# Ranking the second unit of a slot one operation behind the first, in a fused attention and feed-forward kernel

## The chip, the cores and the metric

The kernel runs on one core of a Trainium2 chip. The metric is the device time of one execution in microseconds; the median of three runs before the change is 1221.03 us (1220.47 to 1221.56).

## The reference

Attention that keeps, for each query, only the scores that reach the 32nd largest, then two feed-forward layers of different kind on the result. Batch 4, 8 heads, 576 tokens, 64 dimensions a head; 2304 tokens of 512 features, 2048 hidden.

```python
scores = scale * q @ k^T                       # 4 x 8 x 576 x 576
kth = the 32nd largest of each row
scores = where(scores >= kth, scores, -1e9)
attn = exp(scores - max); attn = attn / (sum(attn) + 1e-9)
x = (attn @ v), heads side by side             # 2304 x 512
h = x @ w_in                                   # first layer
g = h where h >= 1, 0 where h <= -1, else (h + 1)^2 / 4
x = g @ w_out
h = max(x @ w_in2, 0)                          # second layer
out = (h * h) @ w_out2
```

## The kernel before

Attention is cut into units: one head's 128 queries against all 576 keys. Two units make a slot `n`, t = 0 and t = 1 (two heads of the same rows); slots 0 to 63 hold the full blocks, 64 to 71 the packed tails. Matmuls of float32 accuracy are made of three with rounded halves: a value is split into a rounded part (`hi`, by ScalarE) and a rest (`lo`, by GpSimd or VectorE).

A unit goes through the engines in this order. TensorE makes its scores (`score`, L605) and ScalarE copies them to one of four buffers `s_sb` (`copy_scores`, L814), which waits until the masked product of four units before is made. VectorE ranks (`rank`, L1080): four MAX8 (L1086), each giving the next eight largest, with three MATCH_REPLACE8 (L1088) between that strike them out; `RANK_OPS` is 7. ScalarE negates the maxima of both units in one instruction (`negate`, L822) and makes the exponentials (`exponentiate`, L835). The mask comes from the 32nd value: in slots below `SIGNED` = 9 ScalarE makes it with two sign instructions (`keep_by_sign`, L853 and L856), later GpSimd (L1270); GpSimd multiplies it with the exponentials (L1275). TensorE turns the product (`turn_main`, L632), ScalarE copies it (`copy_main`, L863, `copy_shared`, L868), TensorE multiplies by v (`times_v`, L654 and L659) with a column of ones that gives the sum. VectorE takes the sum two slots later (`add_to_total`, L1094) and inverts it (L1104); ScalarE or VectorE scales the result into `x_nat` (L877).

Each engine runs a list of instructions that is written out by hand, slot by slot, and in order. In slot `n` ScalarE has first the signs of slot n-1, then the negation and first exponential of slot n, the scores of slot n+1 and turned tiles of slot n-1 between the two exponentials and behind them, and at the end the rounding of weight blocks for the next slot (`split_ahead`, L801). GpSimd has the products of slot n-1, then the rest of a preparation (`split_kq`, L1253), then weight blocks (L1261). VectorE has for each of the seven operations the first unit and then the second, with other work at fixed operations.

A preparation splits k and q of a pair of heads: SP loads it (L389), ScalarE rounds it into `kq_hi` (L793), GpSimd makes `kq_lo` (L1253), and SP stores both to DRAM (`restack`, L397), from where the slots load `ks` and `qs` (L402, L409). `PREP_SLOT` puts them in slots 1, 3, 5, 7, then 10, 12, 14, 16 and later. Up to slot 17 ScalarE's rounding stands ahead of the second exponential; the loads that SP has in its list behind a `restack` or a weight block wait with it.

The feed-forward work fills TensorE in steps at positions q = 3n, 3n+1, 3n+2: an up product (L700), the curve in three ScalarE instructions and one of VectorE (L1149), the split into `g_hi` and `g_lo` (L974, L977, L1288), a down product (L728, L734) two positions later. It starts at position 31, in slot 10; slots 10 to 17 (`SINGLE`) have two steps, later ones three. After slot 73 only feed-forward work is left.

One semaphore, `rank_step`, counts the rank operations of both units, two per operation.

Of the kernel before, what the change touches and what calls it, by code (L numbers as in the profile page):

```python
# [187 lines left out]
def build(nc, kq, kq0, vv, w_raw, out):  # L188
# [8 lines left out]
    with ctx:  # L197
# [64 lines left out]
        s_copied = sem("s_copied")  # L262
        rank_step = sem("rank_step")
        negated = sem("negated")
# [523 lines left out]
        def _(act):  # L788
# [28 lines left out]

            def negate(n):
                act.wait_ge(rank_step, 2 * RANK_OPS * n + 2)
                if n >= 2:  # L820
                    act.wait_ge(exp_done, 2 * n - 2)
                act.activation(neg_max[n % 2][:, :], top[n % 2][:, :, 0], ACT.Copy,  # L822
                               scale=-SCALE).then_inc(negated, 1)

            def exponentiate(n, t):
                i = (2 * n + t) % 4
                if t == 0:
                    act.wait_ge(negated, n + 1)
                    if n >= 2:
                        act.wait_ge(main_turned[1], n - 1)  # L830
                        act.wait_ge(shared_turned, n - 1)
# [15 lines left out]
            def keep_by_sign(n, t):  # L847

                u = 2 * n + t
                s = s_sb[u % 4]  # L850
                act.wait_ge(exp_done, u + 1)
                act.wait_ge(rank_step, 2 * RANK_OPS * (n + 1) - 1 + t)
                act.activation(s[:, :], s[:, :], ACT.Sign, bias=top[n % 2][:, t, TOPK - 1:TOPK],  # L853
                               scale=-1.0).then_inc(below, 1)
                act.wait_ge(below, u + 1)
                act.activation(s[:, :], s[:, :], ACT.Sign, bias=1.0, scale=-1.0).then_inc(keep_done, 1)  # L856
# [157 lines left out]
            def slot(n):  # L1014
# [13 lines left out]
                if here:  # L1028
                    negate(n)
                    exponentiate(n, 0)  # L1030
# [7 lines left out]
                if n in PREP_SLOT and n in SINGLE:  # L1038
                    hi_at(q)
                if n in SINGLE or q < UP_POS[0]:  # L1040
                    split_new(n)
                if here:
                    exponentiate(n, 1)
                if n in SCALED and n not in SINGLE:
# [9 lines left out]
                copy_at(q + 1)  # L1054
                hi_at(q + 1)
                split_ahead(n)
                if n > SINGLE[-1]:
# [18 lines left out]
        def _(dve):  # L1076
            def rank(n, t, op):
                i, done = (2 * n + t) % 4, op // 2
                src = s_sb[i] if done == 0 else rest[t]
                if op == 0:  # L1080
                    dve.wait_ge(s_copied, 2 * n + t + 1)
                else:
                    dve.wait_ge(rank_step, 2 * RANK_OPS * n + 2 * (op - 1) + t + 1)
                best = top[n % 2][:, t, 8 * done:8 * done + 8]
                if op % 2 == 0:
                    dve.max(best, src[:, :]).then_inc(rank_step, 1)  # L1086
                else:
                    dve.match_replace(rest[t][:, :], best, src[:, :], LOWEST).then_inc(rank_step, 1)  # L1088

# [100 lines left out]
            def slot(n):  # L1190
                here, past = n < SLOTS, 0 <= n - 2 < SLOTS and n - 2 not in SOON

                def both(op):
                    if here:
                        rank(n, 0, op)
                        rank(n, 1, op)

# [11 lines left out]
                for op in (2, 3, 4, 5, 6):  # L1209
# [6 lines left out]
                    if op == 4:  # L1216
                        read_at(3 * n + 1)
                        if n >= DEFERRED[0]:
                            activate_at(3 * n + 1)
                    if here:  # L1220
                        rank(n, 0, op)
                        if op == 2 and n in SINGLE:
                            invert_total(n - 2)
                        rank(n, 1, op)
                    if op == (3 if n in SINGLE and n - 1 in PREP_SLOT else 2):
# [24 lines left out]
        def _(pool):  # L1250
# [13 lines left out]
            def mask(n, t):  # L1264
                u = 2 * n + t
                s, pr = s_sb[u % 4], prob[n % 2]
                pool.wait_ge(exp_done, u + 1)
                pool.wait_ge(rank_step, 2 * RANK_OPS * (n + 1) - 1 + t)
                if n >= SIGNED:
# [121 lines left out]
```

## Time and profile before

| | |
|---|---|
| median of three runs | 1221.03 us (1220.47 to 1221.56) |
| profiled execution | 1220.98 us, span 1219.2 us |
| TensorE busy | 1174.0 us, 96% |
| VectorE busy | 833.0 us, 68% |
| ScalarE busy | 784.0 us, 64% |
| GpSimd busy | 740.3 us, 61% |

The shares are means over unlike stages. The first ten slots have no feed-forward work; the last third of the time has no attention. The span is counted from the first to the last instruction; the execution's time has some more around it.

### The profile page before, as it was taken

How to read it: one execution, taken by the hardware profiler on the slowest of the kernel's cores; microseconds unless marked ns; L12 is line 12 of the kernel's file. 1: busy time of each engine (PE TensorE's matmuls, PEld its weight loads, DVE VectorE, ACT ScalarE, POOL GpSimd, SP SyncE). 2: the span in 40 equal slices, each digit the busy share in tenths (PEclk: the TensorE clock that was granted, in tenths of full speed). 3: DMA queues.
4: the chain of work that ended last, by engine and by line, in shares of the span. 5: the costliest groups of instructions: out<-in, count | busy, mean ns of one | idle time of the engine just before them, and what ended most of it. 6: DMA issues, size and time to landing. Idle time of an engine off the chain costs nothing.

```text
span 1219.2 us, 22952 instructions
## 1 busy us (share of the span) xinstructions
PE 1174.0 (96%) x8120; PEld 1089.9 (89%) x8120; DVE 833.0 (68%) x1847; ACT 784.0 (64%) x1704; POOL 740.3 (61%) x589
## 2 busy tenths in 40 slices
PE   5878999999999999999999999999999999999998
PEld 3777899999889999999999999998999888998887
DVE  7999999999988799999999987878830211110000
ACT  7887777787656767767676665666554544653343
POOL 6777887888877677677776766666742222222222
PEclk9957999999999999999999999999999999999999
DMA  6777897678869923433458831567449400870000
GB/s 252 266 267 252 282 360 295 251 268 315 302 253 393 379 75 109 147 121 112 140 208 297 294 112 41 130 173 183 109 160 361 167 1 1 338 318 1 1 35 18
DMA packets 93377, 237.34 MB, mean 195 GB/s; under 512 B 10320, under 2 KB 45136, under 8 KB 80976
## 3 DMA queue, kind: packets, MB, share of 16 engines
q1 hardware_dynamic: 93104, 235.62, 54.9%
q8 instruction: 65, 1.06, 0.4%
q14 instruction: 48, 0.39, 0.1%
q10 hardware_dynamic: 160, 0.26, 0.1%
HBM read 164.02 MB, written 71.83 MB: 193 GB/s over the span
## 4 chain that ended last, share of the span: by engine, by line
PE 74%; DVE 9%; POOL 8%; ACT 4%; issue 3%; DMA 1%; SPq 0%; ACTq 0%; POOLq 0%; DVEq 0%
PE h_ps L700 22%; PE y_ps L728 11%; PE y_ps L734 10%; PE pv_ps L659 6%; PE score_ps L700 6%; DVE top L1086 5%; PE tr_ps L632 4%; DVE rest L1088 4%; PE score_ps L605 3%; POOL s_sb L1270 3%; POOL prob L1275 2%; POOL kq_lo L1253 2%; PE y_ps L720 2%; PE y_ps L723 2%; PE tr_ps L720 2%
## 5 line engine op out<-in xcount | busy, mean ns | idle before, releaser
L700 PE MATMUL h_ps<-xt_ks,w_in 128*128 128x256 f32 (+1 forms) x2628 | 384.5, 296 | 2.3 <-ACT rg L961 1.6
L700 PEld LDWEIGHTS h_ps<-xt_ks,w_in 128*128 128x128 f32 x2628 | 342.1, 191 | 12.8 <-ACT rg L961 2.0
L1288 POOL TENSOR_TENSOR g_lo<-rg,g_hi 128x256 fp32r<-128x256 f32 x224 | 169.4, 756 | 270.4 <-ACT g_hi L974 153.6
L1086 DVE MAX8 top<-rest 128x8 f32<-128x576 f32 x432 | 305.1, 746 | 0.4
L1270 POOL TENSOR_SCALAR s_sb<-s_sb,top 128x576 f32<-128x576 f32 x126 | 221.5, 1758 | 31.3 <-DVE top L1086 31.3
L1088 DVE MATCH_REPLACE8 rest<-top,rest 128x576 f32<-128x576 f32 x288 | 211.5, 741 | 0.0
L1275 POOL TENSOR_TENSOR prob<-s_sb,prob 128x576 f32<-128x576 f32 x128 | 182.9, 1431 | 16.3 <-ACT s_sb L856 3.5
L728 PE MATMUL y_ps<-g_hi,w_out 128*128 128x256 f32 x896 | 181.4, 285 | 0.6 <-POOL g_lo L1288 0.5
L734 PE MATMUL y_ps<-w_out,g_hi 128*128 128x512 f32 x448 | 158.5, 395 | 1.0 <-ACT moves L935 0.8
L728 PEld LDWEIGHTS y_ps<-g_hi,w_out 128*128 128x128 f32 x896 | 147.5, 191 | 2.1 <-POOL g_lo L1288 1.0
L659 PE MATMUL pv_ps<-v_sb,pt 128*128 128x65 f32 x1024 | 133.6, 288 | 0.0
L659 PEld LDWEIGHTS pv_ps<-v_sb,pt 128*128 128x128 f32 x1024 | 132.1, 209 | 0.0
L728 PE MATMUL y_ps<-g_lo,w_out 128*128 128x256 f32 x448 | 126.7, 283 | 0.0
L814 ACT ACTIVATE s_sb<-score_ps 128x576 f32<-128x576 f32 x143 | 92.1, 644 | 42.2 <-PE score_ps L605 23.4
L1086 DVE MAX8 top<-s_sb 128x8 f32<-128x576 f32 x144 | 102.4, 744 | 12.8 <-ACT s_sb L814 12.7
L632 PE MATMUL tr_ps<-ident,prob 128*128 128x128 f32 x576 | 93.6, 288 | 14.5 <-POOL prob L1275 14.2
L1088 DVE MATCH_REPLACE8 rest<-top,s_sb 128x576 f32<-128x576 f32 x144 | 105.7, 740 | 0.1
L1149 DVE SCALAR_TENSOR_TENSOR rg<-rg 128x256 f32<-128x256 f32 x112 | 59.5, 531 | 62.3 <-ACT rg L967 62.0
L835 ACT ACTIVATE prob<-s_sb,neg_max 128x576 f32<-128x576 f32 x128 | 99.4, 777 | 2.1
L734 PEld LDWEIGHTS y_ps<-w_out,g_hi 128*128 128x128 f32 x448 | 84.5, 189 | 17.7 <-issue 1.4
L956 ACT ACTIVATE rg<-h_ps 128x256 f32<-128x256 f32 x99 | 37.9, 383 | 88.9 <-PE h_ps L700 88.8
L605 PE MATMUL score_ps<-xt_ks,qs_g 128*128 128x288 f32 x480 | 90.9, 314 | 3.0 <-DMA qs_g<-kq_scratch 1.5
(117 smaller groups left out, 1821.8 us busy)
## 6 DMA issues: line engine op xcount, KB each, us to landing
w_in<-w_scratch SPq DMA_DIRECT2D x32, 1024.0 KB, 7.1
w_out<-w_scratch SPq DMA_DIRECT2D x32, 1024.0 KB, 8.4
xt_ks<-kq_scratch SPq DMA_DIRECT2D x30, 576.0 KB, 7.2
w_scratch<-w_in SPq DMA_DIRECT2D x16, 1024.0 KB, 7.2
w_scratch<-w_out SPq DMA_DIRECT2D x16, 1024.0 KB, 6.7
v_sb<-in_vv_dram SPq DMA_DIRECT2D x48, 325.0 KB, 6.1
qs_g<-kq_scratch SPq DMA_DIRECT2D x120, 128.0 KB, 4.3
moves<-in_w_dram SPq DMA_DIRECT2D x27, 512.0 KB, 5.9
```

The source lines that it names most:

```text
L605: last = pe.matmul(score_ps[:, 512 * half:512 * half + HALF], qq[:, t, var, :], kk[:, t, HALF * half:HALF * (half + 1)], start=(var == 0), ...
L632: last = pe.transpose(tr_ps[t][:, P * j:P * (j + 1)], prob[n % 2][:, base + P * j:base + P * (j + 1)], ident[:, :])
L659: last = pe.matmul(pv_ps[:, V1 * t:V1 * (t + 1)], pt[:, base + P * j:base + P * (j + 1)], vb[:, V1 * (2 * j + t):V1 * (2 * j + t + 1)], st ...
L700: last = pe.matmul(h_bank(k), wi[:, f // 2, w, m, cols], x_part(k, x, m), start=(m == 0 and n == 0), stop=(m == KT - 1 and n == 2))
L728: last = pe.matmul(y_ps[i][:, CHUNK * (m % 2):CHUNK * (m % 2 + 1)], wo[:, f // 2, w, f % 2, P * m:P * (m + 1)], g[f % 2][:, :], start=(f = ...
L734: last = pe.matmul(y_ps[i][:, :], g[f % 2][:, P * i:P * (i + 1)], wo[:, f // 2, w, f % 2, :], start=(f == 0 and n == 0), stop=(f == FT - 1 ...
L835: act.activation(pr[:, SEQ * t:SEQ * (t + 1)], s_sb[i][:, :], ACT.Exp, bias=bias[:, t:t + 1], scale=SCALE).then_inc(exp_done, 1)
L1086: dve.max(best, src[:, :]).then_inc(rank_step, 1)
L1088: dve.match_replace(rest[t][:, :], best, src[:, :], LOWEST).then_inc(rank_step, 1)
L1270: pool.tensor_scalar(s[:, :], s[:, :], top[n % 2][:, t, TOPK - 1:TOPK], None, ALU.is_ge).then_inc(keep_done, 1)
L1275: pool.tensor_tensor(pr[:, cols], s[:, :], pr[:, cols], ALU.mult).then_inc(masked, 1)
L1288: pool.tensor_tensor(lo_of(k), u_of(k), hi_of(k).bitcast(F32), ALU.subtract).then_inc(g_lo_done, 1)
```

## The change

- VectorE: the second unit's operation `op` - 1 stands where its operation `op` stood; its last operation stands behind the first operation of the next slot's first unit.
- `rank_step` becomes two semaphores, one for each unit, and all that wait for it wait for their unit's.
- ScalarE: `negate` works on one unit, 128x1 instead of 128x2. That of the second unit stands just ahead of the second exponential, and both exponentials wait for theirs.
- ScalarE: in slots 1, 3, 5 and 7 `split_new` (the rounding of a preparation) moves from ahead of the second exponential to the end of the slot, ahead of `split_ahead`. In slots 10 to 17 it stays.

```diff
-        rank_step = sem("rank_step")
+        rank_step = [sem(f"rank_step{i}") for i in range(2)]
...
-            def negate(n):
-                act.wait_ge(rank_step, 2 * RANK_OPS * n + 2)
+            def negate(n, t):
+                act.wait_ge(rank_step[t], RANK_OPS * n + 1)
                 if n >= 2:
                     act.wait_ge(exp_done, 2 * n - 2)
-                act.activation(neg_max[n % 2][:, :], top[n % 2][:, :, 0], ACT.Copy,
+                act.activation(neg_max[n % 2][:, t:t + 1], top[n % 2][:, t, 0:1], ACT.Copy,
                                scale=-SCALE).then_inc(negated, 1)
 
             def exponentiate(n, t):
                 i = (2 * n + t) % 4
+                act.wait_ge(negated, 2 * n + t + 1)
                 if t == 0:
-                    act.wait_ge(negated, n + 1)
...
                 if here:
-                    negate(n)
+                    negate(n, 0)
                     exponentiate(n, 0)
...
-                if n in SINGLE or q < UP_POS[0]:
+                if n in SINGLE:
                     split_new(n)
                 if here:
+                    negate(n, 1)
                     exponentiate(n, 1)
...
                 copy_at(q + 1)
                 hi_at(q + 1)
+                if n < SINGLE[0]:
+                    split_new(n)
                 split_ahead(n)
...
-                def both(op):
+                def first(op):
                     if here:
                         rank(n, 0, op)
-                        rank(n, 1, op)
+
+                def second(op):
+
+                    if op and here:
+                        rank(n, 1, op - 1)
+                    if op == 0 and 0 <= n - 1 < SLOTS:
+                        rank(n - 1, 1, RANK_OPS - 1)
+
+                def both(op):
+                    first(op)
+                    second(op)
...
-                    if here:
-                        rank(n, 0, op)
-                        if op == 2 and n in SINGLE:
-                            invert_total(n - 2)
-                        rank(n, 1, op)
+                    first(op)
+                    if op == 2 and n in SINGLE:
+                        invert_total(n - 2)
+                    second(op)
```

## Rows read from the trace of the kernel before

**Rows 1.** Busy time by stretch: PE, PEld, DVE, ACT, POOL, granted clock, DMA share, GB/s.

```profile
0.00:107.25 107.25, 80.30 (x319) 65.70 (x320) 98.03 (x216) 89.64 (x155) 77.25 (x46) 0.82 0.75 264
107.25:193.45 86.20, 80.53 (x635) 77.44 (x634) 84.95 (x194) 63.02 (x146) 71.70 (x51) 0.97 0.84 312
...
193.45:1219.20 1025.75, 1013.13 (x7170) 946.77 (x7168) 649.96 (x1439) 631.37 (x1404) 591.39 (x494) 1.00 0.51 177
...
77.95:97.49 19.54, 15.45 (x71) 14.04 (x70) 19.54 (x46) 18.43 (x34) 15.68 (x10) 0.63 0.76 277
```

**Rows 2.** Chain of waits, 76 to 106 us: shares by line.

```profile
by line: DVE top L1086 52.8%; DVE rest L1088 46.1%; DVE total L1094 0.6%; DVE recip L1104 0.6%
```

**Rows 3.** Timeline of ScalarE, slots 5 to 7: start, length, instruction [idle before].

```profile
65.97 1.21 ACT L793 ACTIVATE kq_hi<-kq_lo 128x1216 fp32r<-128x1216 f32 x1
67.08 0.77 ACT L835 ACTIVATE prob<-s_sb,neg_max 128x576 f32<-128x576 f32 x1
...
69.30 1.09 ACT L801 ACTIVATE w_out<-moves 128x1024 fp32r<-128x1024 f32 x1
...
71.20 0.81 ACT L853 ACTIVATE s_sb<-s_sb,top 128x576 f32<-128x576 f32 x1
...
74.01 0.19 ACT L822 ACTIVATE neg_max<-top 128x2 f32<-128x2 f32 x1
74.23 0.78 ACT L835 ACTIVATE prob<-s_sb,neg_max 128x576 f32<-128x576 f32 x1
74.91 0.63 ACT L814 ACTIVATE s_sb<-score_ps 128x576 f32<-128x576 f32 x1
75.58 0.60 ACT L863 ACTIVATE pt<-tr_ps 128x512 f32<-128x512 f32 x1
...
83.92 0.65 ACT L814 ACTIVATE s_sb<-score_ps 128x576 f32<-128x576 f32 x1 [0.74 <-POOL prob L1275]
...
90.43 0.81 ACT L853 ACTIVATE s_sb<-s_sb,top 128x576 f32<-128x576 f32 x1
```

**Rows 4.** Waits, 7 to 107 us: us in total, times, longest.

```profile
POOL kq_lo L1253 <- ACT kq_hi L793: 11.0, 4, 4.2
...
DVE top L1086 <- ACT s_sb L814: 8.7, 4, 7.1
```

**Rows 5.** Timeline of VectorE, slot 6: the second unit's first MAX8.

```profile
68.83 0.76 DVE L1086 MAX8 top<-s_sb 128x8 f32<-128x576 f32 x1 [0.94 <-ACT s_sb L814]
```

**Rows 6.** Timeline of ScalarE, end of slot 14.

```profile
161.27 0.28 ACT L868 ACTIVATE pt<-tr_ps 128x128 f32<-128x128 f32 x1
161.75 0.42 ACT L977 ACTIVATE g_hi<-rg 128x256 fp32r<-128x256 f32 x1 [0.21 <-DVE rg L1149]
```

**Rows 7.** Timeline of GpSimd, products of slot 1, then slots 5 and 6.

```profile
30.72 2.78 POOL L1275 TENSOR_TENSOR prob<-s_sb,prob 128x576 f32<-128x576 f32 x2 [0.58 <-ACT s_sb L856]
...
67.26 2.76 POOL L1253 TENSOR_TENSOR kq_lo<-kq_lo,kq_hi 128x1216 fp32r<-128x1216 f32 x1 [4.15 <-ACT kq_hi L793]
69.98 2.37 POOL L1261 TENSOR_TENSOR w_in<-moves,w_in 128x1024 fp32r<-128x1024 f32 x1
72.89 2.80 POOL L1275 TENSOR_TENSOR prob<-s_sb,prob 128x576 f32<-128x576 f32 x2 [0.54 <-ACT s_sb L856]
```

**Rows 8.** Timeline of TensorE: transposes, products with v, slots 6 and 8.

```profile
74.49 1.05 PE L632 MATMUL tr_ps<-ident,prob 128*128 128x128 f32 x4
...
79.24 3.52 PE L659 MATMUL pv_ps<-v_sb,pt 128*128 128x65 f32 x16
...
98.07 1.90 PE L659 MATMUL pv_ps<-v_sb,pt 128*128 128x65 f32 x16
```

**Rows 9.** Timeline of SP's issues, slots 3 and 4, and of TensorE's scores.

```profile
51.80 0.33 SPq L466 DMA_DIRECT2D moves<-in_w_dram  x1
...
57.38 1.24 SPq L409 DMA_DIRECT2D qs_g<-kq_scratch  x2
...
63.29 1.30 PE L605 MATMUL score_ps<-xt_ks,qs_g 128*128 128x288 f32 x4 [1.51 <-DMA qs_g<-kq_scratch]
```

More of the change, by code:

```diff
@@ L851, in keep_by_sign @@
                 act.wait_ge(exp_done, u + 1)
-                act.wait_ge(rank_step, 2 * RANK_OPS * (n + 1) - 1 + t)
+                act.wait_ge(rank_step[t], RANK_OPS * (n + 1))
                 act.activation(s[:, :], s[:, :], ACT.Sign, bias=top[n % 2][:, t, TOPK - 1:TOPK],
@@ L1082, in rank @@
                 else:
-                    dve.wait_ge(rank_step, 2 * RANK_OPS * n + 2 * (op - 1) + t + 1)
+                    dve.wait_ge(rank_step[t], RANK_OPS * n + op)
                 best = top[n % 2][:, t, 8 * done:8 * done + 8]
                 if op % 2 == 0:
-                    dve.max(best, src[:, :]).then_inc(rank_step, 1)
+                    dve.max(best, src[:, :]).then_inc(rank_step[t], 1)
                 else:
-                    dve.match_replace(rest[t][:, :], best, src[:, :], LOWEST).then_inc(rank_step, 1)
+                    dve.match_replace(rest[t][:, :], best, src[:, :], LOWEST).then_inc(rank_step[t], 1)
             def add_to_total(n):
@@ L1267, in mask @@
                 pool.wait_ge(exp_done, u + 1)
-                pool.wait_ge(rank_step, 2 * RANK_OPS * (n + 1) - 1 + t)
+                pool.wait_ge(rank_step[t], RANK_OPS * (n + 1))
                 if n >= SIGNED:
```

## The prediction

> **What bounds the kernel now.** I read the busy time by stage first, then the chain of waits, then the waits by pair of engines, and last the engines' own rows of the stage that mattered. The reader is to see three stages in [rows 1]: slots 0 to 9 (to 107.25 us), where VectorE is busy 98.03 of 107.25 us; slots 10 to 17, where it is busy 84.95 of 86.20; and the rest, where TensorE is busy 1013.13 of 1025.75. So from 193 us on TensorE sets the pace, and whatever the first ten slots win or lose moves the end by as much, unless the middle stage takes it up. In slots 7 and 8 VectorE is busy 19.54 of 19.54 us, which is the length of its two slots, and the chain of waits there is VectorE's ranking alone [rows 1, 2].
>
> But ScalarE is no more than a breath behind. From its mask of slot 5 (71.20) to that of slot 7 (90.43) its stream takes 19.23 us, of which only 0.74 is a wait of any length [rows 3]. VectorE has to wait for its score copies in slots 3, 4 and 6 (the largest, 0.94 us, at 68.83; 8.7 us with the 7.1 of the start [rows 4, 5]). What is added to ScalarE's stream here is not hidden.
>
> **The change part by part.**
>
> *Ranks of the second unit two operations later.* No operation is added: 14 a slot as before, and the first unit's keep their places, also against the activations and sums between them. Pairs of dependent operations still have one other between them. The second unit's scores are needed about 1.4 us later, its threshold comes about 1.4 us later. The stalls of slots 3, 4 and 6 (8.7 less 7.1, so 1.6 us in all) could go [rows 4, 5]. The late threshold costs nothing: GpSimd masks the first unit for 3.2 us before it takes up the second, and ScalarE, which makes the masks in the slots below 9, reaches the signs of slot 5 at 71.20, when VectorE is long in slot 6 (68.83). Bounds: -2.1 (all of VectorE's idle time to 107.25: 107.25 - 98.03 - 7.1) to 0; I count none by itself, as the next edit decides.
>
> *Negation per unit.* One more ACTIVATE per slot, in ScalarE's queue just ahead of the second exponential, which must wait for it. Price: from the start of the negation to that of the exponential, 74.23 less 74.01 = 0.22 us, 0.45 for two slots [rows 3]. The row shows 0.19 us for the narrow instruction and no overlap with its reader. The Trainium skill (ScalarE: Activation LUTs, section What ACT_TABLE_LOAD costs) gives 186 ns plus 0.833 ns per element and an overlap of about 93 ns back to back; the duration agrees, but here a semaphore stands between. By an estimate from that page, with the overlap, two slots would pay about 0.2 us and not 0.45. In slots 10 to 17 the cover is ScalarE's wait for VectorE ahead of the rounding at 161.75: without the wait it would have begun 0.18 us after 161.27 (0.28 less the 0.1 by which neighbours overlap), so there are 0.3 us against 0.22 [rows 6]. If this is gone a slot pays 0.1, under 1 us for the stage. In the rest TensorE is idle 12.6 us for all reasons together [rows 1], so 0, at most +1.
>
> *Rounding of the preparations (slots 1, 3, 5, 7) at the slot's end.* I take slot 5 as pattern. In ScalarE's own stream this is only an exchange: copy, exponential and turned tiles come 1.11 us earlier (65.97 to 67.08 in [rows 3]), the weight block follows as before. But everything behind the rounding is later. Its new start is where the weight block began, less its own 1.11 and plus one negation: 69.30 - 1.11 + 0.22 = 68.41, so 2.44 later than 65.97. GpSimd's queue is in order: kq_lo, then a weight block, then the masks of the slot. By [rows 7] kq_lo starts 1.29 after kq_hi, the block 2.72 after that, and the mask could start 2.34 after that (2.37 less an overlap): 6.35 in all. Before, that was 72.32, and the mask began at 72.89 because it waited for ScalarE; there are only 0.57 us of cover. Now it is 68.41 + 6.35 = 74.76, and the masked product is ready 1.4 us later: 76.16. Behind it stands ScalarE's copy of the scores (it reuses the s_sb buffer). ScalarE arrives there at 74.91 + 0.22 = 75.13 and waits 1.1 us, counting the semaphore. TensorE's transposes of that unit also start with the product and take 1.05 [rows 8]: the copy of the turned tile could start 0.55 behind the score copy and now waits 0.5 more; before it started at 75.58, 0.67 behind, so it waited 0.15. I take 0.35.
>
> Sum for two slots: 0.45 + 1.1 + 0.35 = 1.9 us. ScalarE's stream goes from 19.23 to 21.1 us, while VectorE needs 19.54. There are four such pairs: 4 x 1.9 = 7.6, less the 0.3 by which ScalarE was ahead of VectorE's pair: +7.3.
>
> A walk through the queues from slot 1 gives the same size. Slot 1 delays kq_lo by 3.4 us (kq_hi also moves behind a score copy that waits for TensorE), the mask of slot 1 from 30.72 [rows 7] to 33.5, VectorE's slot 4 by 1.4 (through pv, whose transposes wait for that mask), slot 6 by about 3.5, slot 8 by 5.8, slot 10 by 7 to 9 us; these are my estimates from the same pitches. SP's queue is passed too. At the end of slot 3 it waits for GpSimd's weight block (51.80), and behind this wait stand the restack, the ks, v and qs loads of slot 6; qs goes out at 57.38, and TensorE already waits 1.51 us for it at 63.29 [rows 9]. With kq_lo over 3 us later all these go out as late; TensorE is by then late itself, so I count no extra for it (to +1.5).
>
> What the first part wins (2.1 at most) is inside this: VectorE no longer waits for the second unit's copy, but for pv and the first copies, which come from the slower loop.
>
> In slots 10 to 17 the roundings stay where they are. The loop there runs from VectorE's last activation of a slot over GpSimd's g_lo and masks, TensorE and pv to the next sum; the first unit's operations and the activations keep their places, so I count 0.
>
> The profiled execution was 1220.98 us, its span 1219.2, with 1.8 around it; the median of the three runs was 1221.03, so the sum carries over: 1221.0 + 7.3 = 1228.3.
>
> TensorE's clock is in this. In 77.95 to 97.49 the granted clock is 0.63 on average, between the levels of 1.2 and 2.4 GHz; the sixteen pv matmuls take 3.52 us at 79.24 and 1.90 at 98.07 [rows 1, 8]; in those slots TensorE is busy 15.45 of 19.54 us. More idle time in each slot speaks for the lower level. The Trainium skill (TensorE: Matmul & The Clock Gate, What's actually happening) says the same, that the default state is throttled and activity releases it; by it the pv pieces would stay at 3.5 us and the time at 1228, and with activity enough for the upper level all through it would be the first rival's.
>
> **Rivals.**
>
> *At the upper clock level.* If the slower slots bring pv down to 1.9 us in most of them, the 0.74 wait and the 0.35 go: 19.23 - 0.74 + 0.45 + 1.1 = 20.0 a pair, 0.5 over VectorE, four times 2, and 1 us more from the start: 1224. For it: the records show both levels already. Against it: more idle time.
>
> *The cover is larger than I think.* GpSimd sits idle 11.0 us in front of the four kq_lo, up to 4.2 [rows 4]. If ScalarE's stream has slack that I don't see (its copies are needed 2 us later by the first unit, 1.4 more by the second), two of the four roundings cost nothing, and the 1.6 us of stalls go: 7.3/2 - 1.6 gives +2, with another slot hidden 0: 1221 to 1223.
>
> *Faster: VectorE is the only bound.* Place: VectorE's first operations of slots 3, 4 and 6, and the sum of pv in slots 10 to 16. If the second unit's slack decides, the roundings behind the slot's copies help by 1.11 us in addition, and the masks don't reach the score copy. This decides if the mask of slot 5 starts before 73.7 (75.13 less 1.4), that is if kq_lo ends a microsecond earlier than by my rows. All of VectorE's idle time in slots 0 to 17 less the start is 2.1 + 1.25 = 3.4 us: 1217.6. For it: the chain of 76 to 106 us is VectorE alone [rows 2]. Against: 0.57 us of cover under a move of 2.4.
>
> That the change doesn't do what it says: the second unit's results come where promised, by the order of the queue; only the stalls may be others.
>
> **The numbers.** Forecast (1225.5 to 1232.5 by itself) 0.5; upper clock level (1223.5 to 1225.5) 0.17; larger cover 0.2; faster 0.13. A change under 0.2% (2.4 us) is not told from none. So faster 0.13, same 0.2, slower 0.67. The range reaches from near the third rival's 1217.6 to the walk's 9 us with SP's 1.5 and ScalarE's 1 in part: 1218.3 to 1232.0.
>
> **What would show it.** Right: VectorE's slot 10 starts 7 us later than 107.25; kq_lo of slot 5 starts over 2.4 us later; GpSimd no longer waits for ScalarE ahead of the masks of slots 1, 3, 5, 7, and ScalarE waits about 1 us for them at its score copy; VectorE waits for pv in slots 3 to 7; from 193 us on all rows are moved by one amount. Wrong: VectorE without idle time in slots 1 to 9; pv at 1.9 us there; or more idle time in TensorE after slot 18, which would mean that the negation or the late threshold costs there.

## The result, and the profile after

The changed kernel takes 1232.22 us (median of six runs, 1231.57 to 1233.3), the kernel before 1221.07 (median of six in the same comparison): 11.2 us slower by the medians; the ratio, which goes by the means, is 1.0088 [1.0075, 1.0101]. Forecast were 7.3. The profiled execution took 1231.57 us, its span is 1229.7, with 1.9 around it; against 1220.98 and 1219.2 that is 10.6 and 10.5 us. The direction and the main mechanism were forecast, the size was too small by 3.9 us, and the time lies on the upper end of the range (0.2 above 1232.0 as it stands; 1.0088 times 1221.03 is 1231.8). In "after" the added ScalarE instructions are visible in the first lines of the page:

```profile
PE 1173.0 (95%) x8120; PEld 1088.1 (88%) x8120; DVE 829.9 (67%) x1847; ACT 797.3 (65%) x1776; POOL 739.9 (60%) x589
```

ScalarE has 72 instructions more (1776 against 1704) and 13.3 us more of busy time, which is 0.18 for each; the other engines have the same counts. Busy time by stretch of the kernel after, the columns as in [rows 1]:

```profile
0.00:114.00 114.00, 77.04 (x313) 61.90 (x313) 97.93 (x215) 91.40 (x164) 77.01 (x46) 0.83 0.69 246
...
114.00:202.07 88.07, 82.43 (x639) 79.42 (x640) 84.79 (x195) 64.67 (x155) 71.49 (x51) 0.95 0.84 308
...
202.07:1229.70 1027.63, 1013.54 (x7170) 946.77 (x7168) 647.15 (x1440) 641.21 (x1458) 591.39 (x494) 1.00 0.51 177
...
82.18:102.57 20.39, 15.04 (x73) 13.12 (x71) 19.63 (x45) 18.38 (x34) 15.38 (x9) 0.58 0.72 259
```

The stretches end at the same work as those of [rows 1]. Slots 0 to 9 are 6.75 us longer, slots 10 to 17 1.87, the rest 1.88. VectorE did the same work in the first stretch (97.93 against 98.03), so the 6.75 are idle time of VectorE. Its slots 1 to 3 start 0.8 us early, mainly because one rank operation of the second unit is still owed at each start. Slot 4 starts 1.2 us late, slot 6 3.3, slot 8 5.1, slot 10 6.75, and slot 11 8.55, as VectorE waits 1.95 us at 119.94, in slot 10, for pv of slot 8. Slots 7 and 8 take 20.39 us, where they took 19.54.

Where it waited now, 7 to 114 us (total, times, longest):

```profile
POOL kq_lo L1265 <- ACT kq_hi L793: 22.8, 4, 7.3
PE tr_ps L632 <- POOL prob L1287: 15.8, 7, 4.8
DVE top L1089 <- ACT s_sb L814: 11.6, 7, 7.1
...
ACT s_sb L814 <- POOL prob L1287: 4.7, 5, 1.0
PE score_ps L605 <- DMA qs_g<-kq_scratch: 4.7, 2, 3.8
DVE total L1097 <- PE pv_ps L659: 4.4, 4, 1.7
```

GpSimd stood 11.0 us ahead of the four kq_lo [rows 4] and now stands 22.8. VectorE's waits for score copies were to shrink by the first part; they grew from 8.7 to 11.6, and 4.4 for pv came to them. One round of this is seen in the timelines of slots 5 to 7. First GpSimd (start, length, instruction, idle before):

```profile
74.85 2.78 POOL L1265 TENSOR_TENSOR kq_lo<-kq_lo,kq_hi 128x1216 fp32r<-128x1216 f32 x1 [7.29 <-ACT kq_hi L793]
...
79.92 2.78 POOL L1287 TENSOR_TENSOR prob<-s_sb,prob 128x576 f32<-128x576 f32 x2
```

kq_lo starts 7.6 us after the 67.26 of [rows 7], in a slot that is itself some 3 us late. The product (second row, behind a weight block of 2.37 us) had its first mask from ScalarE at 78.0 (77.36 and 0.68 in the next fence), and starts at 79.92: the wait for ScalarE that stands in brackets in [rows 7] is gone, and GpSimd comes late by its own queue. ScalarE in the same slots:

```profile
73.53 1.24 ACT L793 ACTIVATE kq_hi<-kq_lo 128x1216 fp32r<-128x1216 f32 x1
...
76.53 0.79 ACT L853 ACTIVATE s_sb<-s_sb,top 128x576 f32<-128x576 f32 x1
77.36 0.68 ACT L856 ACTIVATE s_sb<-s_sb 128x576 f32<-128x576 f32 x1
...
81.36 0.65 ACT L814 ACTIVATE s_sb<-score_ps 128x576 f32<-128x576 f32 x1 [1.03 <-POOL prob L1287]
...
82.59 0.60 ACT L863 ACTIVATE pt<-tr_ps 128x512 f32<-128x512 f32 x1 [0.59 <-PE tr_ps L632]
83.09 0.19 ACT L822 ACTIVATE neg_max<-top 128x1 f32<-128x1 f32 x1
83.31 0.78 ACT L835 ACTIVATE prob<-s_sb,neg_max 128x576 f32<-128x576 f32 x1
...
96.82 0.80 ACT L853 ACTIVATE s_sb<-s_sb,top 128x576 f32<-128x576 f32 x1
```

The score copy waits 1.03 us for the masked product, the turned tile 0.59 for the transposes, and the negation (128x1, 0.19 us) adds 0.22 to its exponential. From sign to sign (76.53 to 96.82) the stream takes 20.3 us, before 19.23 [rows 3]. The chain of waits of the kernel after shows the loop whole; before it was VectorE alone [rows 2] (start, length, what held the end):

```profile
79.92 1.42 POOL prob L1287
81.47 1.10 PE tr_ps L632 x4
...
83.09 0.20 ACT neg_max L822
...
84.92 0.60 ACT pt L863
...
85.69 0.95 ACT w_out L801
86.63 0.67 ACT s_sb L853
87.33 0.69 ACT s_sb L856
88.18 1.43 POOL prob L1287
```

Masked product, transposes, negation, copies, rounding of a weight block, signs, masked product: 8.26 us from the products of slot 5 to those of slot 6, and none of the ranks among these steps. SP's queue passes the delay on (SP's issues, then TensorE's scores):

```profile
56.59 0.33 SPq L466 DMA_DIRECT2D moves<-in_w_dram  x1
...
62.06 1.25 SPq L409 DMA_DIRECT2D qs_g<-kq_scratch  x2
...
68.39 1.30 PE L605 MATMUL score_ps<-xt_ks,qs_g 128*128 128x288 f32 x4 [3.79 <-DMA qs_g<-kq_scratch]
```

The load of weight block 10 went out at 56.59 instead of 51.80 and qs behind it 4.7 us later than in [rows 9]; TensorE waited 3.79 us for it, before 1.51.

### The profile page after: what moved, and what is told of

Same layout as the page of the kernel before. It is cut to its first block, busy times and chain, and to the rows that moved or that the text cites. A ratio compares the mean times of both kernels' runs of the same rounds, so it can differ in the third digit from the quotient of the medians.

```text
span 1229.7 us, 23094 instructions
## 1 busy us (share of the span) xinstructions
PE 1173.0 (95%) x8120; PEld 1088.1 (88%) x8120; DVE 829.9 (67%) x1847; ACT 797.3 (65%) x1776; POOL 739.9 (60%) x589
## 4 chain that ended last, share of the span: by engine, by line
PE 69%; POOL 14%; issue 6%; ACT 6%; DVE 2%; DMA 2%; SPq 1%; ACTq 0%; POOLq 0%
PE h_ps L700 20%; PE y_ps L734 10%; PE y_ps L728 9%; PE score_ps L700 6%; PE pv_ps L659 5%; POOL s_sb L1282 5%; POOL prob L1287 4%; PE tr_ps L632 3%; PE score_ps L605 3%; POOL g_lo L1300 2%; POOL kq_lo L1265 2%; PE y_ps L720 2%; PE y_ps L723 2%; PE tr_ps L723 2%; PE tr_ps L720 2%
## 5 line engine op out<-in xcount | busy, mean ns | idle before, releaser
L1089 DVE MAX8 top<-rest 128x8 f32<-128x576 f32 x432 | 316.2, 746 | 0.4
L659 PE MATMUL pv_ps<-v_sb,pt 128*128 128x65 f32 x1024 | 131.0, 285 | 0.0
L659 PEld LDWEIGHTS pv_ps<-v_sb,pt 128*128 128x128 f32 x1024 | 129.4, 205 | 0.0
L1089 DVE MAX8 top<-s_sb 128x8 f32<-128x576 f32 x144 | 107.8, 749 | 11.6 <-ACT s_sb L814 11.6
L632 PEld LDWEIGHTS tr_ps<-ident,prob 128*128 128x128 f32 x576 | 73.6, 150 | 34.7 <-issue 27.7
```

The lines of the kernel that those rows point to most:

```text
L632: last = pe.transpose(tr_ps[t][:, P * j:P * (j + 1)], prob[n % 2][:, base + P * j:base + P * (j + 1)], ident[:, :])
L659: last = pe.matmul(pv_ps[:, V1 * t:V1 * (t + 1)], pt[:, base + P * j:base + P * (j + 1)], vb[:, V1 * (2 * j + t):V1 * (2 * j + t + 1)], st ...
L1089: dve.max(best, src[:, :]).then_inc(rank_step[t], 1)
```

## The experiments

The kernel before was timed again in each of three groups: 1221.03 us (e1 to e4), 1221.33 (f1 to f4) and 1221.91 (g1 to g4), 27 runs each. Times below are set against the median of the same group; the three differ by 0.9 us, so a difference of that size says little. "Shift" is how much later than in the profile of before TensorE does the same work, found by pairing its 8120 matmuls in order; it is given once slot 10 is past and at the end of the span.

**e1: the kernel after with the rounding back in its place.**

```diff
-                if n in SINGLE:
+                if n in SINGLE or q < UP_POS[0]:
                     split_new(n)
...
                 hi_at(q + 1)
-                if n < SINGLE[0]:
-                    split_new(n)
                 split_ahead(n)
```

> The changed kernel with the rounding of the preparations in slots 1 to 7 back ahead of the second exponential; ranks one operation behind and negation per unit kept. Theory A (the late rounding, through GpSimd's in-order queue, makes the loss of the first ten slots): kq_hi of slot 5 is back within 0.5 us of 2.4 earlier relative to the slot, GpSimd waits for ScalarE's signs again ahead of the masks of slots 1, 3, 5, 7, slot 10 of VectorE starts between 106 and 108 us (107.25 before, 114.00 with the change), and of the 11 us 8 to 9 go: 1221 to 1224, with the 1.9 us that TensorE's part of the changed kernel lost behind slot 18 still there. Rival B (the ranks of the second unit two operations later, or the second negation, make it): slot 10 starts at 111 or later and the time stays over 1227.

Measured: 1223.85 us, ratio 1.002 [1.0011, 1.0029], inside theory A's range; slot 10 starts at 108.61, 0.6 above it. Shift 1.35 us behind slot 10, 3.6 at the end. So three quarters of the 11.2 are the late rounding (with the other two parts present), and the rest grows mostly behind slot 18.

**e2: the kernel before with the late rounding alone.** The semaphore for each unit is kept, the ranks stand as before, one negation for both.

```diff
-                if n in SINGLE or q < UP_POS[0]:
+                if n in SINGLE:
                     split_new(n)
...
                 hi_at(q + 1)
+                if n < SINGLE[0]:
+                    split_new(n)
                 split_ahead(n)
```

> The kernel before with the late rounding alone: both units' ranks side by side, one negation for both. Theory A: the rounding costs 1.1 + 0.35 us at each of four pairs of slots, and the second unit's copies, which now are needed 1.4 us earlier than in the changed kernel, add nothing, as they come 1.1 earlier by the move: 1226.5 to 1229, slot 10 at 113 to 115. Nothing is lost behind slot 18 (under 0.5 us). Rival B: 1221 to 1223. Rival C (the three edits make it worse only together): under 1224.

Measured: 1229.27 us, ratio 1.0064 [1.005, 1.0078], 8.2 us slower by itself. Shift 8.45 and 8.3: nothing more is lost behind slot 10. Its waits, 7 to 116 us:

```profile
PE tr_ps L632 <- POOL prob L1288: 21.0, 5, 4.9
...
DVE top L1092 <- ACT s_sb L814: 15.5, 7, 7.2
```

The second unit's scores are needed earlier here, so VectorE waits 15.5 for copies (11.6 after). But it waits less for pv (1.6, where after has 4.4 and the 1.95 of slot 10), and slot 11 starts 8.46 late against 8.55: the late ranks move the waits from one place to another and win nothing beside the late rounding.

**e3: the kernel after, GpSimd's weight block ahead of kq_lo in slots 1 to 9.** The rounding is as late as after, but the wait for it stands behind the 2.4 us of the block.

```diff
+                if n < SINGLE[0]:
+                    for i in new_blocks(n):
+                        split_w(i)
                 if n in PREP_SLOT and n not in SINGLE:
                     split_kq(PREP_SLOT.index(n))
-                for i in new_blocks(n):
-                    split_w(i)
+                if n >= SINGLE[0]:
+                    for i in new_blocks(n):
+                        split_w(i)
```

> The changed kernel, but in slots 1 to 9 GpSimd takes the weight block ahead of kq_lo. The rounding is as late as in the changed kernel; only what stands between it and the next masks on GpSimd is shorter by a weight block (2.33 us). Theory A: the masks of slots 1, 3, 5, 7 are then ready before ScalarE comes to the copy that waits for them (6.35 less 2.33 = 4.0 us behind kq_hi, and ScalarE's signs of the slot end 4.5 behind it): the 1.0 us waits at the score copies are gone, and SP's wait at the end of slot 3 ends 3 us earlier too: slot 10 at 107 to 109, 1222 to 1225. Rival B (the ranks or the negation): no change from 1232. Rival D (SP: the restack and what stands behind it): the restack is no earlier than in the changed kernel, so ks and qs stay late; slot 6 starts as late as 70.5 and the time stays over 1227.

Measured: 1223.02 us, ratio 1.0014 [1.0005, 1.0023]: 9.2 of the 11.2 us are gone. GpSimd in slot 6:

```profile
68.49 2.79 POOL L1265 TENSOR_TENSOR kq_lo<-kq_lo,kq_hi 128x1216 fp32r<-128x1216 f32 x1 [2.91 <-ACT kq_hi L793]
...
71.84 2.80 POOL L1287 TENSOR_TENSOR prob<-s_sb,prob 128x576 f32<-128x576 f32 x2 [0.57 <-ACT s_sb L856]
```

The product waits for ScalarE's mask again (0.57), not for GpSimd's own queue. Slot 10 starts 0.9 us earlier than before, at 106.32 (expected were 107 to 109); the 1.8 lost behind slot 18 remain. In e1, with the rounding early and the block behind kq_lo, slot 10 starts 2.3 us later than here, so the block's new place may win something of its own; it was not run with the early rounding.

**e4: late ranks alone,** the roundings as before, one negation that waits for both maxima.

```diff
-            def negate(n):
-                act.wait_ge(rank_step, 2 * RANK_OPS * n + 2)
+            def negate(n, t):
+                if t:
+                    return
+                for x in range(2):
+                    act.wait_ge(rank_step[x], RANK_OPS * n + 1)
...
+                def second(op):
+                    if op and here:
+                        rank(n, 1, op - 1)
+                    if op == 0 and 0 <= n - 1 < SLOTS:
+                        rank(n - 1, 1, RANK_OPS - 1)
```

> The kernel before with the second unit's ranks one operation behind alone: one negation for both units, which waits for both maxima, and the rounding where it was. Theory A: the stalls of VectorE in slots 3, 4 and 6 go and nothing else changes: 1219 to 1221; behind slot 18 the same as before within 0.5 us, which puts the 1.9 us of the changed kernel there on the second negation. Rival B (late thresholds hurt the masks): 1223 or more, with TensorE idle longer ahead of the transposes behind slot 18.

Measured: 1222.88 us, ratio 1.0016 [1.0007, 1.0025]: missed. The gain in the first ten slots is there (slot 10 starts 1.3 us early, shift -1.3; 0.66 of it is the operation that VectorE still owes, as f2 shows), and 2.5 us are lost behind slot 18, half of it from 267 to 301 us. The one negation waits for a maximum that comes two operations later, and everything behind it in ScalarE's queue waits too. Not all of the loss is seen to come from this: TensorE waits 1.26 us (0.61 before) at 288.12 for a curve that stands behind the rounding of a weight block, and this had waited 1.90 us for its load.

**f1: the second negation alone,** ranks and rounding as before.

```diff
-            def negate(n):
-                act.wait_ge(rank_step, 2 * RANK_OPS * n + 2)
+            def negate(n, t):
+                act.wait_ge(rank_step[t], RANK_OPS * n + 1)
...
                 if here:
+                    negate(n, 1)
                     exponentiate(n, 1)
```

> The kernel before with the negation per unit alone: ranks side by side and the rounding where it was. After the first runs I hold: the second negation costs its 0.22 us in ScalarE's queue wherever TensorE waits for ScalarE or for what ScalarE feeds behind slot 18, 1.9 to 2.3 us in all there (what ranks and negation together lost there), and 0.45 a pair in the slots up to 9, where ScalarE is as slow as VectorE: slot 10 at 108.5 to 109.5. So 1223.5 to 1225.5. Rival (the late ranks make the loss behind slot 18): as before behind slot 18, 1221 to 1223.

Measured: 1224.08 us, ratio 1.0024 [1.0015, 1.0034]: missed, not in size but in place. Slot 10 starts at 107.33, 0.08 later than before, and the whole 2.6 us of shift come behind slot 18. TensorE's waits there, first before (193 to 1220 us), then f1 (193 to 1222):

```profile
PE tr_ps L632 <- POOL prob L1275: 4.2, 7, 1.1
...
PE h_ps L700 <- ACT rg L956: 0.8, 2, 0.6
PE y_ps L734 <- ACT moves L935: 0.8, 2, 0.7
```

```profile
PE tr_ps L632 <- POOL prob L1283: 4.4, 8, 1.1
PE h_ps L700 <- ACT rg L956: 1.6, 2, 1.2
...
PE y_ps L734 <- ACT moves L935: 1.1, 2, 0.7
```

TensorE waits 0.8 and 0.3 longer for two of ScalarE's results. That is 1.3 with the transposes, half of what was lost. The other half is found when TensorE's matmuls are paired in order with those of before. In f1, e1, e3, f4 and the kernel after, the distance from one matmul to the next grows at the same eight places, by 0.17 to 0.25 us at each: at 210.6, 274.2, 305.1, 346.2, 618.0, 627.7, 834.5 and 888.1 us of before. One of them, before and then after:

```profile
627.70 1.69 PE L700 MATMUL h_ps<-xt_ks,w_in 128*128 128x256 f32 x12 [0.38 <-ACT rg L961]
```

```profile
637.74 1.70 PE L700 MATMUL h_ps<-xt_ks,w_in 128*128 128x256 f32 x12 [0.62 <-ACT rg L961]
```

The wait grows by 0.24 us, about one negation (0.22). The eight make 1.8 of the 1.9 us that the kernel after loses behind slot 18; f1 has 0.63 more, at 288.1. None of the eight grows in e2, e4 or g1, whose kernels have one negation there.

**f2: late ranks in slots 0 to 9 only,** one negation, roundings as before (the cut is against e4).

```diff
-                    if op and here:
-                        rank(n, 1, op - 1)
-                    if op == 0 and 0 <= n - 1 < SLOTS:
+                    if op == 0 and 0 < n <= SINGLE[0]:
                         rank(n - 1, 1, RANK_OPS - 1)
+                    if n >= SINGLE[0]:
+                        if here:
+                            rank(n, 1, op)
+                    elif op:
+                        rank(n, 1, op - 1)
```

> Ranks of the second unit one operation behind in slots 0 to 9 alone, side by side from slot 10 on; one negation for both; rounding where it was. If the 2.5 us that the ranks alone lost behind slot 18 come from the joint negation, which waits for a second maximum two operations later and holds ScalarE's queue, they are gone, and the 1.35 us won by slot 10 stay: 1219.2 to 1220.2. If they come from elsewhere (another state of the queues on entry to slot 18): 1222 or more.

Measured: 1222.01 us, ratio 1.0007 [0.9998, 1.0015]: missed. The loss behind slot 18 went, as expected (shift 0.9 and 1.0), but the shift behind slot 10 is 2.3 us above that of e4. Of this 0.66 is the edit's own: slot 10 has fifteen rank operations here, the last one of slot 9 and fourteen of its own, and takes 12.20 us where before and e4 have 11.54. It takes 12.20 in f3, g1, g3 and g4 as well, and their expectations leave it out. The other 1.6 us arise in slots 0 to 9, whose code is that of e4. Both kernels from 47 to 107 us, first e4 (columns as in [rows 1]), then f2:

```profile
47.00:107.00 60.00, 42.34 (x222) 37.20 (x222) 59.87 (x135) 55.29 (x102) 49.29 (x26) 0.70 0.75 265
```

```profile
47.00:107.00 60.00, 48.58 (x212) 43.72 (x213) 58.64 (x133) 55.00 (x101) 48.09 (x25) 0.57 0.72 253
```

Six pv pieces took 3.51, 3.52, 3.52, 3.52, 3.18 and 3.51 us in f2 and 2.43, 1.90, 2.61, 1.90, 3.52 and 1.90 in e4. So a single profile of the first slots is uncertain by some 1.6 us where the code is the same. That TensorE's clock is the cause fits these rows, but was not shown by itself.

**f3: f2 with VectorE's sum of pv one operation later in slots 0 to 8.**

```diff
-                behind = 2 if n < SIGNED else 1 if n < UP_POS[0] // 3 else 0
+                behind = 3 if n < SIGNED else 1 if n < UP_POS[0] // 3 else 0
```

> The kernel of f2, and in slots 2 to 8 VectorE takes the sum of pv (and inverts it) one operation pair later. With ranks alone VectorE's only idle time of slots 1 to 9 was 1.37 us ahead of the sum in slot 3 and 0.13 in slot 6. Two rank operations later they are gone: slot 10 at 104.4 to 104.8 and 1217.8 to 1218.8. Rival: the late scaling holds ScalarE and TensorE's next pv, and nothing is won: 1219.5 or more.

Measured: 1221.77 us, ratio 1.0002 [0.9993, 1.001]: missed. Its profile (span 1218.9, slot 10 at 106.02) shows a shift of -0.6, and the waits for pv down to 0.5 us from 3.0 in f2; in the median nothing is left of it.

**f4: the kernel after, weight block 10 loaded later by SP,** so that the loads of k, v and qs no longer stand behind the wait for GpSimd's block.

```diff
+STAGE_SLOT[10] = 4
```

> The changed kernel with all its three parts, but SP issues the load of weight block 10, which waits for GpSimd's weight block behind kq_lo, at the end of slot 4 and not of slot 3, so that the restack and the ks, v and qs loads of slot 6 are not behind it. If part of the first ten slots' loss runs through SP's in-order queue (TensorE waited 3.8 us for qs at 68.39, 1.5 before), that wait shrinks to under 1.5 us and 1 to 3 us are won: 1229.5 to 1231.5. If TensorE is late itself and only GpSimd's masks count, as I predicted (no extra for SP): 1231.7 to 1232.7.

Measured: 1229.09 us, ratio 1.0061 [1.0049, 1.0073], so 3.3 us of the loss came through SP's queue (1.0088 less 1.0061 of 1221), a little more than the 1 to 3 expected. Slot 10 starts at 111.22, 3.97 later than before and 2.8 earlier than after; this profiled execution took 1227.13 us, 2 us under the median of its five. SP and TensorE:

```profile
59.06 1.19 SPq L410 DMA_DIRECT2D qs_g<-kq_scratch  x2
...
65.35 1.30 PE L606 MATMUL score_ps<-xt_ks,qs_g 128*128 128x288 f32 x4 [0.32 <-DMA qs_g<-kq_scratch]
```

qs goes out 3.0 us earlier than after, and TensorE's wait falls from 3.79 to 0.32.

**g1: all three parts in slots 0 to 9 only;** from slot 10 on the ranks and the one negation of before.

```diff
             def negate(n, t):
+                if n >= SINGLE[0]:
+                    if t:
+                        return
+                    for x in range(2):
+                        act.wait_ge(rank_step[x], RANK_OPS * n + 1)
...
+                    if n >= SINGLE[0]:
+                        if here:
+                            rank(n, 1, op)
+                    elif op:
+                        rank(n, 1, op - 1)
```

> The changed kernel with all three parts in slots 0 to 9, and from slot 10 on as before (ranks side by side, one negation for both). The part behind slot 18 (1.9 us in the changed kernel's trace, 2.5 with the negation alone) should be gone, the 8.6 of the first slots should stay: 1229.5 to 1231, TensorE's shift against before constant from slot 13 on within 0.3. If the loss behind slot 18 came from entering it late, it stays: 1232.

Measured: 1232.18 us, ratio 1.0077 [1.0065, 1.009]: the time missed, the place right. Behind slot 10 only 0.6 us are lost (9.9 to 10.6) where the kernel after loses 1.9, but behind slot 10 it is 1.3 later than after, 0.66 of it for the fifteenth rank operation. TensorE's waits for products and for `moves` behind slot 18 are those of before (4.2 and 0.8 us), those for the curve 1.2 instead of 0.8, and none of the eight steps of f1 is there.

**g2: e2 with GpSimd's weight block first (the edit of e3).**

```diff
+                if n < SINGLE[0]:
+                    for i in new_blocks(n):
+                        split_w(i)
                 if n in PREP_SLOT and n not in SINGLE:
                     split_kq(PREP_SLOT.index(n))
```

> The kernel before with the late rounding, and in slots 1 to 9 GpSimd takes the weight block ahead of kq_lo; ranks side by side, one negation for both. If the weight block between kq_lo and the masks (and SP's wait for it) is the whole of the rounding's 8.2 us, this is as before or a little better, since the second unit's copies come 1.1 us earlier: 1219.5 to 1221.5. If the late rounding costs something of its own (restack, ks and qs late): 1223 or more.

Measured: 1220.79 us, ratio 0.9992 [0.9982, 1.0002], shift -0.7 and -0.8. The whole 8.2 us of the late rounding are gone by a change of GpSimd's order alone. As in e3, it is open whether this order wins something of its own.

**g3: f3 with the later load of f4.** Ranks late in slots 0 to 9, sum later, SP's load later; roundings and negation as before.

```diff
+STAGE_SLOT[10] = 4
```

> The kernel of f3 (ranks behind in slots 0 to 9, late sum, rounding early, one negation), with SP's load of weight block 10 at the end of slot 4. VectorE's 0.92 us wait at slot 6 came from qs landing late (TensorE waited for it); it should go: slot 10 about 105 and 1218.5 to 1221. Rival: the next limit (pv or ScalarE) takes its place: 1221.5 or more.

Measured: 1220.03 us, ratio 0.9977 [0.9967, 0.9987]: faster than both kernels, by 1.9 us against the median timed beside it (the kernel after stands at 1.0088). In its first slots VectorE waits for copies only at the start, and 0.5 for pv (7 to 107 us):

```profile
DVE top L1091 <- ACT s_sb L815: 7.1, 1, 7.1
...
DVE total L1099 <- PE pv_ps L660: 0.5, 1, 0.5
```

The shift is -1.6 us up to 250 us. The profiled execution is one of its slower runs (1221.61): from 267 us on its shift is +0.7, for a reason told in the last section.

**g4: f3 with the late rounding and the weight block first.**

```diff
-                if n in SINGLE or q < UP_POS[0]:
+                if n in SINGLE:
                     split_new(n)
...
+                if n < SINGLE[0]:
+                    split_new(n)
...
+                if n < SINGLE[0]:
+                    for i in new_blocks(n):
+                        split_w(i)
```

> Ranks behind in slots 0 to 9, late sum, one negation for both, the rounding late and GpSimd's weight block ahead of kq_lo: every wait of VectorE in slots 1 to 9 that a trace so far showed is taken away, so its ranking alone bounds them: slot 10 at 104.4 to 105.0, 1218.0 to 1219.5, faster than before. Rival (ScalarE's own stream, 18.3 us of work in two slots and its waits, is as long as VectorE's 19.5): slot 10 at 106 or later, 1220.5 or more.

Measured: 1222.67 us, ratio 1.0 [0.9992, 1.0009]: missed. Slot 10 starts at 106.36 (in this profile slot 9 waited 1.98 for pv, which took 3.51 us, TensorE's lower level), and from 267 to 301 us 3.3 us are lost, where TensorE waits 2.41 at 289.64 behind a late load of a weight block. A gain of the late rounding beside the late ranks is thus not seen.

## Why the prediction was right in kind and short in size

- *Late rounding keeps kq_lo and the masks back.* Right. GpSimd no longer waits for ScalarE ahead of the product, ScalarE waits 1.03 to 1.04 us at its score copies at 34.62, 57.95, 81.36 and 101.65, four times, where 1.1 were forecast. The forecast for slot 6 was +3.5 (3.3 measured), for slot 8 +5.8 (5.1), for slot 10 7 to 9 (6.75, with 8.55 in slot 11). That the late rounding is the cause is shown by e1 and e2, and that it acts through GpSimd's order by e3 and g2: with the block ahead of kq_lo the rounding stands as late in ScalarE's queue, and the loss is gone. That the walk came so near is in part luck, as it counted nothing for SP's queue.
- *The pair of slots.* ScalarE's stream was to take 21.1 us and took 20.3. The wait for transposes cost 0.59 - 0.15 = 0.44, not 0.35; the 0.74 of [rows 3] went, since pv ran in 1.90 us in slot 7 (86.08). This is the mechanism of the first rival. The sum also takes ScalarE's 0.3 us of lead off once, where that rival takes it off in each pair; done in each, 4 x (1.9 - 0.3) is 6.4. With SP's part taken away, f4's median is 7.8 us above before, 2.1 of it behind slot 18 by its trace, so some 5.7 are left for the first slots, and its fast profiled execution had slot 10 at +3.97. Both are under 7.3. So the 7.3, which came so near to slot 10's 6.75, was too large for what it counted, and the next point makes up for it: luck, not precision.
- *"I count no extra for it (to +1.5)", of SP's queue.* This step failed: the term was put at nothing, and f4 measures 3.3 us. TensorE was late, as I said, but by 2.8 us where qs was late by 5.1: the scores start at 68.39 instead of 63.29, and the wait ahead of them rose by 2.3 (1.51 to 3.79). SP's list holds the loads of slot 6 behind a wait for GpSimd's weight block, and that block stands behind kq_lo, so the whole delay of kq_lo arrives there undiminished.
- *The second negation behind slot 18, "0, at most +1".* This step failed as well, and its own sign of being wrong, more idle time of TensorE there, came: 1.9 us after, 2.6 in f1, 1.8 in e3. [rows 1] gives 12.6 us of idle TensorE there "for all reasons together", and I read that as cover. It is a sum of moments in which TensorE waits for another engine, and at eight such moments the 0.22 us of ScalarE come through in full, which is 1.8 us; at the others they are covered. e4 shows that a late negation costs as well: one negation, later by two ranks, loses 2.5, in other places (276, 288, 486, 556 and 626 us). The two losses don't add (1.9 after for both).
- *The negation in the first slots, 0.45 a pair.* Not seen by itself: f1 is 0.08 us later at slot 10. ScalarE's stream has more slack against VectorE than the 0.3 a pair that I gave it, as long as the rounding and the ranks are where they were. With the late ranks it may be paid: e1, which differs from e4 by the second negation, starts slot 10 2.7 us later. But pv took 3.5 us in all of e1's slots up to 9 and 1.9 to 2.6 in most of e4's, and the medians differ by 1.0 over the whole kernel, so the negation and TensorE's clock are not separated there, nor were the 0.45 beside the late rounding.
- *Late ranks, "-2.1 to 0".* Their gain is there in slots 0 to 9 (e4: -1.3; g3 with the sum and SP's load: -1.6 behind slot 10, the owed operation paid). Beside the late rounding it is nothing, as counted: VectorE waits 11.6 us for copies where e2 waits 15.5, but more for pv, and at slot 11 both are 8.5 late.

By medians: late rounding alone +8.2, negation alone +2.8, ranks alone with one negation +1.9, ranks and negations +2.8, all +11.2. The first and the fourth sum to 11.0. No rival came true as a whole. The third (VectorE the only bound, 1217.6) is what should be left when both queues are relieved; g3 (1220.03) is the nearest to it. f3 and g4 come out 3 us above their expectations, and their traces show most of it: slot 10 was expected at 104.4 to 105.0, which is a shift of -2.3 to -2.9, and it is -0.6 and -0.2 behind slot 10, with 0.66 for the fifteenth rank operation and, in g4, 1.98 for pv; g4 loses 3.3 more from 267 to 301 us. What stays open: what the medians of f3 have lost beyond its profile (1221.77 against 1220.69), how the losses of e4 come about one by one, and what the block's place ahead of kq_lo is worth with the early rounding.

## What to carry to other kernels

Before an instruction is moved later in an in-order queue, follow its reader through every queue that it stands in: here the rounding was harmless on ScalarE; it cost 8.2 us by itself through GpSimd, where a mask stood behind its reader, and through SP, where loads stood behind that. With all parts in place SP's share was 3.3 us; in e2 it was not separated. Other work put ahead of the waiting reader took away both (e3, g2). And idle time of the bounding engine, summed over a long stretch, is no cover for an instruction added in each round: a 0.2 us operation repeated in each of 72 slots cost 1.8 to 2.6 us of a stretch with 12.6 idle, 1.8 of it at eight moments. And an operation that is moved behind a boundary is still owed there: when the late order ends in slot 10, VectorE pays 0.66 us.

## What was not expected of the hardware

The rate at which TensorE runs in the first ten slots differs between kernels whose code is the same there: the granted clock is 0.70 in e4 and 0.57 in f2 over 47 to 107 us, with TensorE busy 42.34 and 48.58 of 60 us. The levels are 2.4 and 1.2 GHz, pv at 1.90 and 3.52 us. The column of the granted clock is not to be read alone here: in e1 it is 1.00 over the same stretch, though its pv pieces all took 3.51 or 3.52 us.

GpSimd's mask took 1.73 us, but 2.95 and 3.15 where VectorE split a weight block at the same time. g3, GpSimd, then VectorE, then TensorE's two waits:

```profile
247.20 3.15 POOL L1287 TENSOR_SCALAR s_sb<-s_sb,top 128x576 f32<-128x576 f32 x1
...
256.86 1.73 POOL L1287 TENSOR_SCALAR s_sb<-s_sb,top 128x576 f32<-128x576 f32 x1
...
260.80 2.95 POOL L1287 TENSOR_SCALAR s_sb<-s_sb,top 128x576 f32<-128x576 f32 x1
```

```profile
260.66 0.43 DVE L1154 SCALAR_TENSOR_TENSOR rg<-rg 128x256 f32<-128x256 f32 x1
261.02 1.21 DVE L1181 TENSOR_TENSOR w_in<-kq_lo,w_in 128x1024 fp32r<-128x1024 f32 x1
```

```profile
251.98 0.63 PE L633 MATMUL tr_ps<-ident,prob 128*128 128x128 f32 x4 [0.88 <-POOL prob L1292]
...
265.40 0.63 PE L633 MATMUL tr_ps<-ident,prob 128*128 128x128 f32 x4 [0.55 <-POOL prob L1292]
```

The second of these masks began 0.7 us earlier than in the kernel before, and the product behind it 0.5 us later. Behind the two masks TensorE waits for the products, 0.88 and 0.55 us, and a moment later 0.31 for g_lo; the shift goes from -1.6 to -0.6 and then to +0.7. So the whole lead of g3 in its profiled execution was lost at these two masks. 1.73 and 1.21 are 2.94, as if the mask had stood still for all of VectorE's instruction. The Trainium skill (SBUF — State Buffer, Who interferes with whom) says that a VectorE instruction with two SBUF inputs contends with a GpSimd instruction that reads SBUF; this trace agrees. It also says, of VectorE's two-port modes, that whoever issues first gets the shared ports for the whole instruction and the other is blocked, not slowed. Here the mask had begun 0.22 us ahead of the weight block's row and was the one that grew, but another VectorE instruction with two SBUF inputs, the first DVE row, had begun 0.14 us ahead of the mask. And "for the whole instruction" does not hold of the mask. In the kernel before the same two overlapped by 0.78 us (first GpSimd's, then VectorE's row), and neither was longer:

```profile
261.52 1.72 POOL L1270 TENSOR_SCALAR s_sb<-s_sb,top 128x576 f32<-128x576 f32 x1
```

```profile
262.46 1.21 DVE L1176 TENSOR_TENSOR w_in<-kq_lo,w_in 128x1024 fp32r<-128x1024 f32 x1
```

The fourteen traces together hold 57 such pairs of a mask and a split weight block, and they fall into groups by how long after the mask VectorE's instruction began. In 28 it began 0.62 us or more behind the mask's start: the masks took 1.71 to 1.74 us and the weight blocks 1.19 to 1.21, neither longer, with up to 1.1 us of overlap. In five it began 0.42 to 0.49 behind: the mask kept its 1.73, and VectorE's ended 1.82 behind the mask's start, as if it had begun at 0.61. In 15 it began ahead of the mask, and the mask took 2.69 to 2.72, VectorE's 1.38 to 1.82. In the remaining nine, 0.22 to 0.42 behind, another VectorE instruction of two inputs stood just ahead, and the mask took 1.98 to 2.00 in seven and the 2.95 and 3.15 in g3's two. By these rows the mask, when it is first, shuts VectorE out for its first 0.6 us only, and what such a pair costs, from nothing to 1.4 us, depends on some tenths of a microsecond of shift.
